# Spectral filter and mixture of experts on one core: one table, ten unused products, two block turns and the indirect transfers take other places

## The reference

```python
X = np.fft.rfft(x, axis=1)                       # x: 8 x 3072 x 256
y = np.fft.irfft(X * (filt_r + 1j * filt_i)[None], n=3072, axis=1)
x = y.reshape(8 * 3072, 256)
# N, D, E, F = 3072, 256, 8, 1024, capacity 768
logits = x @ w_gate                              # 24576 x 8
expert_idx = np.argmax(logits, axis=1)           # one expert a token
gate_w = softmax(logits)[arange, expert_idx]
# in order of the tokens, the first 768 of each expert are kept
h = np.maximum(np.einsum('ecd,edf->ecf', disp, w1), 0.0)
y = np.einsum('ecf,efd->ecd', h, w2)
out[i] = gate_w[i] * y[expert_idx[i], pos[i]]    # zero for tokens not kept
```

## Time and profile before

| | |
|---|---|
| median of three runs | 571.45 us (571.38 to 573.11) |
| the profiled execution | 565.93 us, its span 564.1 us |
| mean granted TensorE clock over the span | 0.939 of 2.4 GHz |
| PE busy | 473.3 us (84%), 3786 matmuls |
| DVE, ACT, POOL busy | 220.3, 206.2, 216.1 us |
| chain that ended last | PE 64%, DMA 11%, issue 8%, DVE 6%, ACT 5% |

### The profile page before, as it was taken

One profiled execution on the slowest core, in us unless ns is written; L12 is line 12 of the kernel. 1 busy time (PEld: TensorE's weight loads), 2 busy tenths in 40 slices (PEclk: granted clock), 3 DMA queues, 4 the chain that ended last, 5 costly groups with the idle time before them and its releaser, 6 DMA issues.

```text
span 564.1 us, 9447 instructions
## 1 busy us (share of the span) xinstructions
PE 473.3 (84%) x3786; PEld 379.9 (67%) x3786; DVE 220.3 (39%) x335; ACT 206.2 (37%) x362; POOL 216.1 (38%) x190
## 2 busy tenths in 40 slices
PE   5455686899979773788973799999999999999995
PEld 2123242355535441487972799999999999999995
DVE  7034132233355798348600543324433244332220
ACT  2301332454544424425110544434444344443321
POOL 7070100000000000574177318765587655876212
PEclk9859988999999996969986799999999999999998
DMA  8899988988687576999121022963129731193001
GB/s 296 313 355 409 406 285 276 334 261 278 209 271 265 175 226 200 387 401 365 64 75 56 24 99 75 394 250 133 38 76 390 262 131 45 61 380 133 29 21 42
DMA packets 64532, 119.72 MB, mean 212 GB/s; under 512 B 7760, under 2 KB 35296, under 8 KB 64480
## 3 DMA queue, kind: packets, MB, share of 16 engines
q1 hardware_dynamic: 33168, 70.95, 35.6%
q0 software_dynamic: 9824, 25.33, 12.5%
q10 hardware_dynamic: 21488, 22.75, 11.9%
HBM read 60.78 MB, written 58.23 MB: 211 GB/s over the span
## 4 chain that ended last, share of the span: by engine, by line
PE 64%; DMA 11%; issue 8%; DVE 6%; ACT 5%; ACTq 4%; SPq 1%; POOLq 0%; POOL 0%; DVEq 0%
PE back L1257 21%; PE bank L1243 12%; PE wide L1243 11%; PE back L483 5%; DMA u_scratch<-v_out 4%; PE low L516 4%; ACTq L665 3%; PE wide L470 2%; PE low L1226 2%; ACT t_out L658 2%; DMA t_scratch<-t_out 2%; PE bank L531 2%; ACT v_out L672 2%; DVE pq L770 2%; PE low L498 1%
## 5 line engine op out<-in xcount | busy, mean ns | idle before, releaser
L1257 PE MATMUL back<-w2h,hh 128*128 128x256 f32 x384 | 110.5, 288 | 1.0 <-ACT o_out L1028 1.0
L1257 PE MATMUL back<-w2l,hh 128*128 128x256 f32 x384 | 109.4, 285 | 0.0
L1257 PE MATMUL back<-w2h,hl 128*128 128x256 f32 x384 | 109.3, 285 | 0.0
L770 DVE TENSOR_TENSOR pq<-wide,fab 128x1024 f32<-128x1024 f32 x45 | 55.0, 1223 | 118.1 <-PE wide L470 114.8
L1070 DVE SCALAR_TENSOR_TENSOR hl<-wide,hh 128x384 fp32r<-128x384 f32 x64 | 34.8, 555 | 129.0 <-ACT hh L1019 97.6
L1161 POOL DMA_INDIRECT out<-o_out,token x48 | 51.2, 1068 | 83.0 <-ACT o_out L1028 73.9
L1257 PEld LDWEIGHTS back<-w2h,hh 128*128 128x128 f32 x384 | 74.3, 193 | 1.2 <-ACT o_out L1028 1.2
L1257 PEld LDWEIGHTS back<-w2h,hl 128*128 128x128 f32 x384 | 74.4, 194 | 0.0
L1257 PEld LDWEIGHTS back<-w2l,hh 128*128 128x128 f32 x384 | 74.3, 194 | 0.0
L1133 POOL DMA_INDIRECT g_in<-y_rows,token x48 | 51.5, 1073 | 58.6 <-DVE token L932 37.7
L1028 ACT ACTIVATE o_out<-back,o_gate 128x256 f32<-128x256 f32 x48 | 22.7, 475 | 104.6 <-PE back L1257 90.9
(11 more groups left out here) (129 smaller groups left out, 777.0 us busy)
## 6 DMA issues: line engine op xcount, KB each, us to landing
out<-zero SPq DMA_DIRECT2D x24, 1024.0 KB
w_raw<-in_w SPq DMA_DIRECT2D x14, 1024.0 KB
u_scratch<-v_out ACTq DMA_DIRECT2D x48, 192.0 KB, 4.1
t_scratch<-t_out ACTq DMA_DIRECT2D x30, 256.0 KB, 6.6
z_in<-t_scratch SPq DMA_DIRECT2D x24, 256.0 KB, 3.9
x_in<-in_x POOLq DMA_DIRECT2D x12, 512.0 KB, 14.1
x_in<-in_x SPq DMA_DIRECT2D x6, 512.0 KB, 6.3
z_in<-t_scratch SPq DMA_DIRECT2D x24, 128.0 KB, 5.1
```

Of the source, the lines that this page charges most:

```text
L770: nc.vector.tensor_tensor(pq[:, n % 3], spectrum(t, h)[:, :, 0, :].unsqueeze(2).to_broadcast([P, 2, 2, D]), fab[:, h], ALU.mult).then_inc( ...
L1257: mm = nc.tensor.matmul(ps[4 + (b * ST + s) % 2][:, 0:D], hx[:, b % 2, f, s * P:(s + 1) * P], wt[:, k, f, :], start=(f == 0 and m == 0), s ...
```

## The change

- **Table first.** `pe_last` does the table of the second batch ahead of the first step of the way back instead of after step 2. VectorE makes `token[0]` directly behind it, ahead of expert 0's low part and the clearing of the zeros.
- **Unused products.** Ahead of that table TensorE does ten matmuls of the identity with a constant tile, 128x384, into a free bank. Nothing reads them.
- **Block turns.** Block 0 is turned in `pe_last` behind step 6 (its `xh` and `xl` move with it, the latter behind the low part of expert 1's first weights). Block 1 is turned inside up 0, in front of group `TURN_AFTER = 6`, with its `xh` and `xl` in the same place of ScalarE's and VectorE's order.
- **Results of block 1.** ScalarE does the first two ahead of block 2's `xh`, the third behind it, instead of all three behind it.
- **Indirect transfers.** A new helper `pool_after` makes GpSimd wait until TensorE has done some up groups. The order is now: gather 0, low part for expert 0, gather 1, (5 groups of block 0) gates 0, low part for expert 1, gate store, gates 1; scatter 0, gather 2, scatter 1, gather 3, (6 groups of block 2) gates 2, (2 of block 3) gather 4, (7 of block 3) gates 3; then gather 5, scatter 2, gates 4, gates 5, and on as before.

Left out below are the parts for a second round, which isn't run here.

```diff
+TURN_AFTER = 6
-NEXT_TABLE = 2
+UNUSED = 10
...
+        def pe_block_turn(pe, r, b):
+            n = number(r, b)
+            pe.wait_ge(g_loaded[b % 2], (n // 2 + 1) * 16 * ST)
+            if n > 0:
+                pe.wait_ge(xl_done, n * DH)
+            for h in range(DH):
+                for s in range(ST):
+                    mm = nc.tensor.transpose(ps[h][:, s * P:(s + 1) * P], g_in[:, b % 2, s, h * P:(h + 1) * P], ident)
+                mm.then_inc(gt_done, 1)
+
-        def pe_last(pe, t):
+        def pe_last(pe, t, r):
             pe.wait_ge(v_evac, (t + 1) * NG)
+            if r == 0:
+                pe.wait_ge(m_done, (t + 1) * NH)
+                for _ in range(UNUSED):
+                    nc.tensor.matmul(ps[2][:, 0:3 * P], ident, sq[:, :, :], start=True, stop=True)
+            pe_table(pe, t - 1, 4)
             for i in range(span(t)):
                 pe_tokens(pe, t, i, t + 1, True, t - 1)
-                if i == NEXT_TABLE:
-                    pe_table(pe, t - 1, 4)
+                if r == 0 and i == products(t):
+                    pe_block_turn(pe, r, 0)
...
         def act_last(act, t, r):
...
                 act_tokens(act, t, i, True, False)
+                if r == 0 and i == products(t):
+                    act_block_turned(act, r, 0)
...
         def dve_last(dve, t, r):
             for n in range(NEXT_STEPS[-1], HOT):
                 dve_route(dve, t - 1, n, 7)
+            for n in range(HOT, ROUTE_STEPS):
+                dve_route(dve, t - 1, n, 4)
+            if r == 0:
+                dve_tokens(dve, t - 1, 0)
+                nc.vector.tensor_scalar(least[:, 1:2], least[:, 0:1], 2.0, None, ALU.mult).then_inc(flag_set, 1)
+            low_split(dve, r, 0, 0)
             if r == 0:
                 dve.wait_ge(bi_done, (t + 1) * NG)
                 nc.vector.memset(zero[:, :], 0.0).then_inc(zero_set, 1)
-            low_split(dve, r, 0, 0)
-            for n in range(HOT, ROUTE_STEPS):
-                dve_route(dve, t - 1, n, 4)
-            if r == 0:
-                nc.vector.tensor_scalar(least[:, 1:2], least[:, 0:1], 2.0, None, ALU.mult).then_inc(flag_set, 1)
-                dve_tokens(dve, t - 1, 0)
             dve.wait_ge(w_loaded[0], (r * (E - 1) + 1) * 16)
             dve.wait_ge(w1h_done, r * E + 1)
             nc.vector.tensor_copy(w1h[:, 1].rearrange("p h f -> p (h f)"), raw_of(1, 0)).then_inc(w1h_done, 1)
             low_split(dve, r, 1, 0)
+            if r == 0:
+                dve_block_turned(dve, r, 0)
...
             def upped(b):
...
                 for f in range(FT):
+                    if b == 0 and f == TURN_AFTER:
+                        turned(1)
                     act.wait_ge(h_done, n * FT + f + 1)
...
+            act_exp(act, last - 1)
             if r > 0:
-                act_exp(act, last - 1)
-            turned(0)
-            if r == 0:
-                act_exp(act, last - 1)
+                turned(0)
             for b in range(BLOCKS):
...
                 if b == 1:
                     downed(0)
-                if b < BLOCKS - 1:
+                    downed(1, range(2))
+                if 0 < b < BLOCKS - 1:
                     turned(b + 1)
...
                 if b == 1:
-                    downed(1)
+                    downed(1, range(2, ST))
...
+        def pool_after(pool, r, b, f):
+
+            pool.wait_ge(h_done, number(r, b) * FT + f)
+
         def pool_last(pool, t, r):
...
                 pool_gather(pool, r, 1)
+                pool_after(pool, r, 0, 5)
                 pool_gates(pool, r, 0)
-                pool_gates(pool, r, 1)
                 low_split(pool, r, 1, 1)
                 gate_store(pool, t)
+                pool_gates(pool, r, 1)
...
         def pool_experts(pool, r, last):
+            pool.wait_ge(first_zeroed, 16 * FIRST_ZEROS)
...
+            pool_sent(pool, r, 0)
             if r == 0:
                 pool.wait_ge(tokens_set, 6)
                 rows_ready(pool, last)
             pool_gather(pool, r, 2)
+            pool_sent(pool, r, 1)
             pool_gather(pool, r, 3)
-            pool.wait_ge(first_zeroed, 16 * FIRST_ZEROS)
...
-            pool_sent(pool, r, 0)
+            pool_after(pool, r, 2, 6)
             pool_gates(pool, r, 2)
+            pool_after(pool, r, 3, 2)
+            pool_gather(pool, r, 4)
+            pool_after(pool, r, 3, 7)
             pool_gates(pool, r, 3)
-            pool_sent(pool, r, 1)
-            pool_gather(pool, r, 4)
-            pool_gates(pool, r, 4)
             for b in range(2, BLOCKS - 1):
...
                 pool_sent(pool, r, b)
+                if b == 2:
+                    pool_gates(pool, r, 4)
...
             def up(b):
...
+                    if b == 0 and f == TURN_AFTER:
+                        turn(1)
...
-            turn(0)
+                turn(0)
             up(0)
-            turn(1)
             up(1)
```

More of the change, by code:

```diff
@@ L755, in act_last_stage, with act_block_turned @@
             act_back(act, t, NG - 1)
+        def act_block_turned(act, r, b):
+            n = number(r, b)
+            for h in range(DH):
+                act.wait_ge(gt_done, n * DH + h + 1)
+                if h == 0 and n >= 2:
+                    act.wait_ge(h_done, (n - 1) * FT)
+                nc.scalar.copy(xh[:, b % 2, h, :], ps[h][:, 0:TOK]).then_inc(xh_done, 1)
         def act_last(act, t, r):
@@ L811, in dve_last, with dve_block_turned @@
             low_split(dve, r, 1, 0)
+            if r == 0:
+                dve_block_turned(dve, r, 0)
+        def dve_block_turned(dve, r, b):
+            n = number(r, b)
+            for h in range(DH):
+                dve.wait_ge(xh_done, n * DH + h + 1)
+                nc.vector.tensor_tensor(xl[:, b % 2, h, :], ps[h][:, 0:TOK], xh[:, b % 2, h, :].bitcast(F32),
+                                        ALU.subtract).then_inc(xl_done, 1)
         def by_token(a):
@@ L1003, in turned @@
             def turned(b):
[L1004 to L1009, removed]
+                act_block_turned(act, r, b)
             def upped(b):
@@ L1017, in upped, with downed @@
                 for f in range(FT):
+                    if b == 0 and f == TURN_AFTER:
+                        turned(1)
                     act.wait_ge(h_done, n * FT + f + 1)
                     nc.scalar.activation(hh[:, b % 2, f, :], ps[(2, 3, 6, 7)[f % 4]][:, 0:TOK], ACT.Relu).then_inc(hh_done, 1)
-            def downed(b):
+            def downed(b, parts=range(ST)):
                 n = number(r, b)
                 act.wait_ge(gates_loaded[b % 4], (n // 4 + 1) * 16 * ST)
-                for s in range(ST):
+                for s in parts:
                     if n >= 2:
@@ L1061, in turned @@
             def turned(b):
[L1062 to L1066, removed]
+                dve_block_turned(dve, r, b)
             def upped(b, f):
+                if b == 0 and f == TURN_AFTER:
+                    turned(1)
                 dve.wait_ge(hh_done, number(r, b) * FT + f + 1)
@@ L1191, in pool_experts @@
         def pool_experts(pool, r, last):
+            pool.wait_ge(first_zeroed, 16 * FIRST_ZEROS)
+            if r > 0:
+                pool.wait_ge(rest_zeroed, 16 * LATE_ZEROS)
+            pool_sent(pool, r, 0)
             if r == 0:
@@ L1219, in turn @@
             def turn(b):
-                n = number(r, b)
-                pe.wait_ge(g_loaded[b % 2], (n // 2 + 1) * 16 * ST)
-                if n > 0:
-                    pe.wait_ge(xl_done, n * DH)
-                for h in range(DH):
-                    for s in range(ST):
-                        mm = nc.tensor.transpose(ps[h][:, s * P:(s + 1) * P], g_in[:, b % 2, s, h * P:(h + 1) * P], ident)
-                    mm.then_inc(gt_done, 1)
+                pe_block_turn(pe, r, b)
             def up(b):
@@ L1352, in run @@
                 pe_last_stage(pe, last - 1, r, last - 1 > first + 2)
-                pe_last(pe, last - 1)
+                pe_last(pe, last - 1, r)
                 pe_experts(pe, r, last)
```

5 lines of the change are left out of this document (1 added, 4 removed).

## The result

| | before | after |
|---|---|---|
| median of four runs | 571.64 us (571.38 to 573.11) | 551.58 us (550.09 to 553.07) |
| ratio after to before, 95% interval | | 0.9644 (0.9612 to 0.9676) |
| profiled execution, its span | 565.93, 564.1 us | 550.09, 548.3 us |
| mean granted clock, PE busy | 0.939, 473.3 us (3786) | 0.963, 472.4 us (3806) |

3.6% faster, 547.8 predicted. The profiled executions differ by less, 15.8 us, since code that the change leaves alone took other times in them: the last result of the inverse transform was copied out at 213.55 us before and at 219.20 after. In the twelve profiles of the experiments, which share this code, the point lies between 215.8 and 222.3 us. So before's profile was an early one; it also lies 5.7 us under its own median.

The account below looks back on a forecast made before the run. Before a fixed tail of 244.9 us, late tokens, waits for turned rows and ScalarE's stall under 24 transfers bound the kernel. 3.5 + 2.3 + 2.0 + 17.8 - 2.0 = 23.6 us off the 571.45 median gave 547.8, range 537 to 560.

Parts of the forecast that it names:

- What the long row costs: Block 2's up products to block 3's: without ScalarE's lateness under 24 transfers, 28.0 us becomes 10.2, gain 17.8.
- First term: Start of block 0's up products: early table and turn bring them to 240.0 us, gain 3.5, bounds 3 and 6.
- the cast of w1h: VectorE's cast of expert 1's first weights, ahead of block 0: GpSimd's pass holds it until 235.3 us.
- Second term: Block 0's to block 1's up products: the wait for block 1's turn goes, 14.7 us becomes 12.4, gain 2.3.
- The middle stretch: Block 1's up products, block 0's down products and half table: keeps its relative times, no gain or loss.
- Third term: Block 2's turn to its up products: 4.3 us instead of 6.3, gain 2.0.
- The zeros: Clearing that block 0's scatters wait for: done near 262 us, nothing lost if done by 269.
- The new row: Transfers after block 2's up products: eight then seven with a 1 us gap, -2.0 us, bounds 0 and -11.
- The lateness did move: Rival: the new 15 transfers starve ScalarE as the 24 did, 11.1 us instead of 2.0, total 557; chance 0.17.
- No gather ended last: Rival: gathers 2, 3 and 4 land late, delaying turns 2 to 4 by 4, 3 and 2 us, total 557; chance 0.09.
- The clock held: Rival: full clock is not held, ten products last 15.8 us, first term becomes -2.1, total 553; chance 0.06.
- ScalarE caught up: Rival: ScalarE never catches up from 281 to 318 us, adding 32 us, total 580; chance 0.05.

Follow-up runs that it names:

- e1: The changed kernel with GpSimd's order of before, nothing else altered; 565.06 us, ratio 0.9881 to the kernel before.
- e2: The kernel before with only GpSimd's new order and its waits; 559.88 us, ratio 0.981.
- e5: The kernel before plus a VectorE clearing of one column per up group of blocks 2 and 3, on TensorE's signal; 554.34 us, one run, before 553.8.
- e12: The kernel before plus one small VectorE memset per product group of blocks 2 and 3, on a third chip; 553.85 us, ratio 1.0033.
- e10: The changed kernel again, unaltered, on a chip without the stall; 548.77 us against 553.29 before, ratio 0.9899.
- the first comparison: The changed kernel against the kernel before, on a chip not on record; 551.58 us against 571.64, ratio 0.9644.
- e7: The changed kernel with GpSimd gathering gates of block b+2 instead of b+3 from block 2 on; 544.39 us, ratio 0.9841 to before.
- e3: The changed kernel without the ten unused products; 555.6 us, ratio 0.9707 to the kernel before.
- e4: The changed kernel with blocks 0 and 1 turned at their old places; 551.64 us, ratio 0.9638 to the kernel before.
- e11: The changed kernel with gates of b+2, w2's low part ahead of them, expert 1's w2 cast and split early, third chip; 543.66 us, ratio 0.9876.

## Why the prediction was right

- **What the long row costs: 17.3 us measured for 17.8.** e1 and e2 show from both sides that GpSimd's order makes and removes the stall. That it is a lateness of ScalarE which grows with the row stays argued: e5 and e12, which were to tell it from a late signal of TensorE, met no stall. In their traces the same row costs ScalarE nothing, so the row is not enough by itself; what has to be added to it is open. In before's trace nothing but GpSimd's own queue moves data from 291 to 312 us, so a weight load or code load is not it (queue, packets, MB, share of the 16 DMA engines):

```profile
q0 software_dynamic: 624, 0.92, 14.3%
```

- **First term, 3.5 taken, 5.2 measured.** Table at 220.99 on before's scale for 221.5 predicted, tokens 223.28 for 223.8, turn 0 234.29 for 234. The products came near their lower bound (6.72 us, with 6.4 by columns) instead of 7.9. The step that was off is the cast of w1h: I had GpSimd's pass hold it until 235.3; what it waited for was its load, 6.62 us, and it started at 238.35. On before's scale that is 232.7, 2.6 us before the time I gave it. It then took 2.16 us for 1.23 in the earlier trace rows and ended at 240.51, 1.09 behind the end of GpSimd's pass (234.89 + 4.53 = 239.42). By the exclusive lock of the Trainium skill (SBUF — State Buffer, "SBUF: two separate sides") it should stand until that end and then take its 1.23, to 240.65. The trace agrees within 0.14 us; wrong was only what I took to come last in front of it. One working of the term doesn't come out of its own steps: without the lock they give 236.8 (TensorE's 234 + 2.8), so a term of 6.6 and not 5.7, above the stated bound of 6.
- **Second term, 2.3 taken, 3.5 measured** (up 0 to up 1, 14.72 to 11.24). I had taken up 0's clock as before, half for its first 5.9 us. Measured it was half for 3.1 us, and back 3.6 us after up 0's start (243.92 to 247.48); with full clock throughout I had 4.5.
- **The middle stretch was to keep its relative times. It lost 2.3 us** (up 1 to turn 2, 26.74 to 29.04). This is the one step that I left out of the sum. Turn 2 waits in both kernels for gather 2, which waits for the tokens of the half batch at the end of VectorE's routing. In that routing GpSimd's second low part at 257.73 meets VectorE's L913 at 258.54, which takes 3.97 us for 0.35, and TensorE waits 2.51 us at 263.03. Before had the same meeting with L878, 2.67 us, so the port's price rose by 1.3 because VectorE came 0.8 us behind GpSimd's start and not 2.2. The other 1.0 is ScalarE's: its cast of w2h (255.75, 1.90 us) lay in the gap ahead of up 1 before, and now, with the gap gone, it holds back the first result of up 1, so that L913 starts 3.38 us behind up 1's start where L878 started 2.38. I had used the rule for the cast of w1h and not for this pass.
- **Third term, 2.0 taken, 2.8 measured** (6.34 to 3.58). The zeros held scatter 0 for 4.56 us until 272.11, 266.5 on before's scale, where I had estimated 262 and called 269 harmless: gather 2, behind the scatters, waited for its tokens anyway (278.72).
- **The new row, -2.0 taken, -5.0 measured** (tail 244.87 to 249.88), inside the bounds of 0 to -11 and the term furthest off. From turn to turn the loss lies in three places. 0.9 us stand ahead of turn 4, which waits 0.73 for its gather. 1.5 stand from turn 5 to turn 6 (18.10 to 19.59 us), a consequence that I didn't follow: the row ends in three more gates and delays the low part queued behind it, with the load, cast and product behind that. 2.2 stand from turn 13 to turn 15 (35.41 to 37.61 us), where ScalarE is late again, under a row of nine transfers at 492 to 504; the other 0.4 are behind turn 15. The same kernel on the second chip (e10) has the second of these, 19.63 us, and not the third: 35.42 us, with the same row of nine at 492 to 504. ScalarE there in the changed kernel of the first comparison, one of its late copies, where e10 has 0.55 us of idle at 502.30:

```profile
502.34 0.49 ACT L1051 ACTIVATE hh<-bank 128x384 fp32r<-128x384 f32 x1 [2.33 <-PE wide L1274]
```

- **Sum**: 5.2 + 3.5 - 2.3 + 2.8 + 17.3 - 5.0 = 21.5 for 23.6. Of the 3.8 us between 547.8 and 551.58 that is 2.1; the rest, 1.7, is how far the two profiled executions lie from their medians and from each other at the copy. The range's lower end was wider than its terms: with every early term at its best and nothing for the new row they give 540.6, not 537.
- **Rivals.** The lateness did move, in a small form; 15 transfers gave an idle of 2.90 us at 325.85 for 0.55 usual, 2.4 late, and not 15/24 of the stall. No gather ended last for more than 1.7 us, no more than before. The clock held until the table (1.00 from 215 to 225). ScalarE caught up.

What neither prediction nor rivals had: that the price of the long row is not the kernel's alone. It came on the chip at 571.8 and in the first comparison, and not on two others. The runs of each chip lie within minutes of each other, so whether the stall goes with the chip or with the hour isn't shown. On the second chip the change brings 4.5 us (553.29 to 548.77), against 23.6 in my sum; the measured sum without its 17.3 is 4.2. 548.77 is near the time I gave only because the kernel before has no stall there either. So the forecast was right by its mechanism where the stall is; that the changed kernel was measured where it is, was luck.

## What to carry to other kernels

An unbroken row of indirect transfers is worth cutting, but cut it by what stands behind it on GpSimd: three transfers in front of a compute pass that frees a load buffer cost 2.0 us between two turns (e7 against e10). Where a profile shows one engine idle by something it can't name, run the kernel on another chip, and again later, before pricing the idle as part of the kernel. Ask of every GpSimd pass which VectorE step will meet it.

## What the runs showed of the hardware

- One kernel, 571.8 us on one chip (13 runs, 568.9 to 574.9), 553.3 on a second (7 runs) and 552.8 on a third (19 runs). Where the stall is, up 2 to up 3 takes 27.98 us in the kernel before; in the two probes, which are that kernel with a few clearings more, it takes 10.64 and 10.99 on the other two chips. That stretch is 17 of the 18.5 us between the medians. ScalarE has waits put down to "remote" in the six profiles of the first comparison and of the chip at 571.8 (the former perhaps another chip, at the same 571.6), and in none of the eight from the other two. The wait view of ScalarE, the changed kernel of the first comparison and e1 (us in all, number of waits, the longest):

```profile
ACT hh L1051 <- remote: 4.1, 3, 2.2
ACT xh L779 <- remote: 1.5, 2, 0.9
```

```profile
ACT hh L1051 <- remote: 18.1, 3, 7.2
ACT o_out L1060 <- remote: 7.4, 1, 7.4
```

- A VectorE step of 0.17 us took 4.24 and one of 0.35 took 3.97 beside a GpSimd pass of 4.6 us over 128x2048: each ended 0.03 to 0.2 us behind the pass. The cast of w1h meets GpSimd's first pass in nine traces (the changed kernel, e1, e3, e4 and e7 to e11). Alone it takes 1.23 us; there it took from 1.36 (e11) to 3.41 (e3), and in all nine it ended 1.09 or 1.10 us behind the pass.
- After 8.66 us without work TensorE ran at half clock; ten unused products, twenty passes of 128x384, kept it at full clock in the gap and took 6.72 us of a wait. They did not keep it for what follows: in the changed kernel TensorE waited 1.73 us ahead of up 0, and 0.5 us into up 0, at 244.4, the clock fell to half.
- The transform ahead of all this, 213.5 to 222.3 us for the same code, is a wider spread than most of the effects here; stages had to be counted from its end.
